# Second tile's rows loaded ahead, and some of the first tile's products moved to rows 64 to 127

## What is computed

```
w   = softmax(weight_gen) over 7 taps, for each token and each of 8 heads
x1  = sum over 7 taps of w[k] * x[token - 6 + k]       (24 channels to a head)
h1  = x1 @ w_in1 (192 x 2048);   x2 = (max(h1, 0) * h1) @ w_out1 (2048 x 192)
h2  = x2 @ w_in2 (192 x 2048);   out = (h2 * cos(h2)) @ w_out2 (2048 x 192)
```

## Time and profile before

| | value |
|---|---|
| median of three runs | 1176.63 us |
| the profiled execution | 1176.54 us |
| its span, first to last instruction | 1174.7 us |
| TensorE busy | 1167.3 us (99%) |
| VectorE busy | 961.2 us (82%) |
| ScalarE busy | 805.9 us (69%) |
| GpSimd busy | 367.1 us (31%) |
| mean granted TensorE clock | 0.999 of full speed |

### The profile page before, as it was taken

The page is one execution under the profiler, slowest core; times in us unless marked ns, Lnnn a source line. Parts: engine busy times, 40 slices in busy tenths (PEclk is TensorE's granted clock), DMA queues, the critical chain, the costliest instruction groups (busy, mean ns, idle before and its releaser), DMA issues.

```text
span 1174.7 us, 25693 instructions
## 1 busy us (share of the span) xinstructions
PE 1167.3 (99%) x9906; PEld 1129.7 (96%) x9906; DVE 961.2 (82%) x1505; ACT 805.9 (69%) x1467; POOL 367.1 (31%) x265
## 2 busy tenths in 40 slices
PE   9999999999999999999999999999999999999998
PEld 7989999999999999999999999999999999999987
DVE  7968898878778787887878878787787878878787
ACT  5977766666666676666766666676666766666676
POOL 4994634070420606025070430705215070000000
PEclk9999999999999999999999999999999999999999
DMA  8511111110111101111011111101111000100001
GB/s 212 138 48 31 37 27 35 25 35 10 23 35 29 35 11 18 35 28 35 15 24 29 25 35 28 35 9 21 35 29 35 13 17 3 26 2 15 1 1 28
DMA packets 113173, 37.32 MB, mean 32 GB/s; under 512 B 101662, under 2 KB 110878, under 8 KB 113052
## 3 DMA queue, kind: packets, MB, share of 16 engines
q1 hardware_dynamic: 111100, 34.87, 14.3%
q10 hardware_dynamic: 1952, 0.80, 0.3%
HBM read 23.84 MB, written 6.29 MB: 26 GB/s over the span
## 4 chain that ended last, share of the span: by engine, by line
PE 99%; DVE 0%; ACT 0%; ACTq 0%; issue 0%
PE y L608 51%; PE h L608 46%; PE y L713 1%; PE h L637 0%; ACT L1131 0%; PE h L630 0%; PE y L674 0%; DVE tap L1426 0%; PE h L644 0%; PE h L640 0%; ACTq L378 0%; ACTq L389 0%; ACTq L433 0%; PE y L676 0%; PE y L675 0%
## 5 line engine op out<-in xcount | busy, mean ns | idle before, releaser
L608 PE MATMUL y<-g_hi,wo 64*128 64x512 f32 x3048 | 695.1, 393 | 0.2
L608 PE MATMUL y<-g_lo,wo 64*128 64x512 f32 x2032 | 515.9, 391 | 0.0
L608 PEld LDWEIGHTS y<-g_hi,wo 64*128 64x128 f32 x3048 | 414.3, 184 | 14.1 <-PE y L608 1.1
L529 POOL TENSOR_TENSOR tap<-xc,gen 128x768 f32<-128x768 f32 x98 | 151.3, 1550 | 575.4 <-DVE xd_lo L1513 555.3
L608 PEld LDWEIGHTS y<-g_lo,wo 64*128 64x128 f32 x2032 | 298.6, 184 | 1.7
L1167 ACT ACTIVATE turns<-turns 128x512 f32<-128x512 f32 x238 | 150.2, 631 | 182.6 <-DVE turns L1464 182.6
L608 PE MATMUL h<-xa_hi,wa_hi 64*128 64x512 f32 x1018 | 267.6, 397 | 0.1
L608 PE MATMUL h<-xa_hi,wa_lo 64*128 64x512 f32 x1018 | 262.7, 391 | 0.0
L608 PE MATMUL h<-xa_lo,wa_hi 64*128 64x512 f32 x1018 | 262.3, 391 | 0.0
L1484 DVE TENSOR_TENSOR h<-h,turns 128x512 f32<-128x512 f32 x238 | 165.6, 696 | 114.7 <-ACT turns L1167 114.2
L1458 DVE SCALAR_TENSOR_TENSOR h<-h,relu 128x512 f32<-128x512 f32 x249 | 173.4, 696 | 56.5 <-ACT relu L1142 54.3
(11 more groups left out here) (124 smaller groups left out, 1076.0 us busy)
## 6 DMA issues: line engine op xcount, KB each, us to landing
xc<-in_x_dram SPq DMA_DIRECT2D x60, 240.0 KB
out_dram<-arena SPq DMA_DIRECT2D x62, 64.0 KB, 1.9
xt_a<-x_blocks SPq DMA_DIRECT2D x224, 16.0 KB, 1.8
arena<-in_moe_w_out_dram SPq DMA_DIRECT2D x16, 192.0 KB, 3.3
arena<-in_moe_w_in_dram SPq DMA_DIRECT2D x16, 128.0 KB, 2.6
out_dram<-arena SPq DMA_DIRECT2D x62, 32.0 KB, 1.7
xt_d<-x_blocks SPq DMA_DIRECT2D x112, 16.0 KB, 1.8
arena<-in_moe_w_in_dram SPq DMA_DIRECT2D x16, 64.0 KB, 2.9
```

The lines of the kernel that those rows point to most:

```text
L529: pool.tensor_tensor(tap[:, k % 2, :].rearrange("p (r g) -> p r g", g=GROUP), rows[k], wk, ALU.mult).then_inc(pool_step, 1)
L608: return pe.matmul(o, w[rows, :], x[rows, :], start=start, stop=stop)
```

## The change

Six things are edited:

1. SP's `load_rows(1)` stands ahead of `load_gen(sp, 1)`.
2. `CONV_SLOTS` moves the second tile's convolution up: three operations after slot 0, two after slot 1, one after each of slots 2 to 9. `turn_at(0)` goes from slot 13 to slot 12.
3. The three softmax steps that stood after slot 0 now stand ahead of the low parts of x, before slot 0.
4. SP copies the high part of the last 64 channels of x, and for pieces 3 to 7 the matching `wd_lo` and every second 128 columns of `wd_hi`, from rows 0 to 63 to rows 64 to 127, each by a DMA inside the on-chip memory.
5. In slots 6 to 15, `xd_hi*wd_lo` (even slots), or `xd_hi*wd_hi` and `xd_hi*wd_lo` (odd slots), is made on BOTTOM. An even slot then has 10 products on TOP and 9 on BOTTOM, an odd one 9 and 10.
6. In all of slots 3 to 19 the first BOTTOM `up_a` is issued ahead of the first TOP `down_a`, and the last TOP `down_a` is the slot's last product.

```
-        return (SLOTS - 3, SLOTS - 9)[t] if t < PEEL else TURN
+        return (SLOTS - 4, SLOTS - 9)[t] if t < PEEL else TURN
-        CONV_SLOTS = (1, 1, 2, 2, 3, 4, 5, 6, 7, 8, 9, 10, 11)
+        CONV_SLOTS = (0, 0, 0, 1, 1, 2, 3, 4, 5, 6, 7, 8, 9)
-        SOFTMAX_AFTER = {0: [(1, 2), (1, 3), (1, 4)]}
-        SOFTMAX_AFTER.update({n: [(n - 1, 0)] for n in range(3, 10)})
+        SOFTMAX_AFTER = {n: [(n - 1, 0)] for n in range(3, 10)}
+        def moved_down(n):
+            return () if not FIRST_MOVED * PF <= n < SLOTS else (0, 1) if n % 2 else (1,)
...
+            def copy_head_weights(pc):
+                cols, odd = slice(pc * PIECE, (pc + 1) * PIECE), slice(pc * PIECE + P, (pc + 1) * PIECE)
+                sp.wait_ge(piece_ready[pc], 2)
+                for w, at in ((wd_lo, cols), (wd_hi, odd)):
+                    sp.dma_start(w[DD:P, at].bitcast(F32), w[0:DD, at].bitcast(F32)).then_inc(head_w_copied[pc], 16)
...
+            load_rows(1)
             load_gen(sp, 1)
-            load_rows(1)
             for pc in range(RING, RING + 2):
                 load_piece(pc)
+            sp.wait_ge(x1_hi_ready, 2)
+            sp.dma_start(xd_hi[DD:P, 0, :].bitcast(F32), xd_hi[0:DD, 0, :].bitcast(F32)).then_inc(head_x_copied, 16)
             load_gen(sp, 2)
             for pc in range(RING + 2, PL + 4):
                 load_piece(pc)
+                if FIRST_MOVED <= pc - RING + 1 < PL:
+                    copy_head_weights(pc - RING + 1)
...
+            def up_d_bottom(o, f, k, **group):
+                w = wd_lo if k == 1 else wd_hi
+                return half(o, w[:, f * P:(f + 1) * P], xd_hi[:, 0, :], BOTTOM, **group)
...
                 for k in range(3):
                     last = down_a(down, BOTTOM, k, start=k == 0)
-                    last_up = up_d(o, 0, i, par, k)
+                    if k < len(kept):
+                        last_up = up_d(o, 0, i, par, kept[k])
...
+                pe.wait_ge(h1_left, n - HEAD_D1 + 1)
+                up_a(o, 0, i, par, BOTTOM, 0)
                 pe.wait_ge(y1_a_left, downs_in_halves(down_of_slot(n)))
                 down_a(down, TOP, 0)
-                pe.wait_ge(h1_left, n - HEAD_D1 + 1)
-                up_a(o, 0, i, par, BOTTOM, 0)
+                up_a(o, 0, i, par, BOTTOM, 1)
                 down_a(down, TOP, 1)
-                up_a(o, 0, i, par, BOTTOM, 1)
+                last_up = up_a(o, 0, i, par, BOTTOM, 2, stop=not moved)
+                if moved:
+                    pe.wait_ge(head_x_copied, 16)
+                    pe.wait_ge(head_w_copied[i // PF], 32)
+                for k in moved:
+                    last_up = up_d_bottom(o, i, k, stop=k == moved[-1])
+                last_up.then_inc(up1_done, 1)
                 down_a(down, TOP, 2, stop=True).then_inc(down1_done, 1)
-                up_a(o, 0, i, par, BOTTOM, 2, stop=True).then_inc(up1_done, 1)
...
                               ALU.subtract).then_inc(piece_ready[0], 1)
+            for op in range(2, 5):
+                softmax(1, op)
             for part in range(2):
                 dve.wait_ge(x1_hi_ready, part + 1)
```

More of the change, by code:

```diff
@@ L241, in conv_ffn_ffn_kernel @@
         w_copied = sem("w_copied")
+        head_w_copied = [sem(f"head_w_copied{pc}") for pc in range(PL)]
+        head_x_copied = sem("head_x_copied")
         y1_summed = sem("y1_summed")
@@ L250, in conv_ffn_ffn_kernel @@
         LATE = 4
+        FIRST_MOVED = 3
         ACT_SQUARES = (2, 3, 4, 5, 6, 7, 8)
-        CONV_SLOTS = (1, 1, 2, 2, 3, 4, 5, 6, 7, 8, 9, 10, 11)
+        CONV_SLOTS = (0, 0, 0, 1, 1, 2, 3, 4, 5, 6, 7, 8, 9)
         HI_AT = {4: 2, 5: 4, 6: 5, 7: 6, 8: 8, 9: 9, 10: 11, 11: 13, 12: 15, 13: 18, 14: 20, 15: 22}
@@ L1057, in head_slot @@
                 n = SLOTS * t + i
+                moved = moved_down(n)
+                kept = [k for k in range(3) if k not in moved]
                 ups_of_slot(t, i, n, -1)
```

## The result

The changed kernel took **1183.35 us** (median of 6, 1180.97 to 1184.53), the kernel before, beside it, 1176.62 (6 runs, 1176.37 to 1177.24): ratio 1.0054, 95% interval 1.0043 to 1.0065. It is slower by 6.7 us; the forecast was 1176.3, with an upper end of 1177.8. The profiled execution is its fastest, 1180.97 us, span 1179.2, 4.5 us over the span before.

The account below looks back on a forecast made before the run. TensorE held 99% of the chain, with TOP bounding a head slot and VectorE close to the bound up to slot 6. 2.87 + 0.10 - 3.34 = -0.37 us gave 1176.3 us, range 1174.4 to 1177.8.

Parts of the forecast that it names:

- the softmax steps ahead of slot 0: VectorE before x's low parts: scaling step takes one turn behind POOL, x 1.17 us later, TensorE's third product about 1.15.
- Convolution after slots 0 and 1: VectorE's three operations after slot 0 and two after slot 1 delay TensorE; slot 6 starts 2.87 us late, x's delay included.
- Products moved: Slots 6 to 15: TOP loses 15 products, 3.50 us, less 0.16 for lags; gain 3.34 us.
- after slot 16 all follows TensorE: Past the faster slots, everything was taken to shift along with TensorE, carrying the sum of -0.37 us to the end.
- nearly 9 us on: SP's weight copies: first pair due about 35.5, nearly 9 us after POOL makes piece 3's wd_lo; counted 0.
- the rows' order: SP issues the second tile's rows before the softmax inputs: no wait taken, bounds 0 and 0.5 us.
- third rival: Pieces 4 and 5 arrive late, ScalarE waits 2.3 us before relu 3: +1.9 us, 1178.5 (1179.1 with upper delay); chance 0.06.
- the new order in slots 3 to 5: BOTTOM's first up_a earlier, TOP's down_a last: hidden behind TOP, taken as 0, else about 0.1 us a slot.
- ScalarE behind faster slots: Slots 6 to 9: ScalarE falls back 1.1 us against a reserve of about 1.3; cost 0.1 us, bounds 0 and 0.5.
- The second rival (program order): Matmuls start in program order, a pair of slots takes 20.4 products, gain only 1.87 us: +1.1, 1177.7; chance 0.15.
- The first rival: Early stall short: scaling step gets in ahead of POOL, few convolution meetings, delay 0.98 us: -2.3, 1174.4; chance 0.17.

Follow-up runs that it names:

- POOL held: Changed kernel with POOL waiting for the second tile's scaling step before its second operation (wd_lo of piece 1): 1176.67 us, ratio 0.9998.
- the two other kernels whose profiles show 3.54 and 3.57: Kernel before with only the softmax steps ahead of x, 1184.55 us; changed kernel with eight fillers instead of one before slot 0's third product, 1181.62 us.
- the run with 0.83: Kernel before with the products moved, their copies and new order, plus POOL's wait for x2_split before the third tile's second convolution product: 1176.12 us, ratio 0.9992.

## Why the prediction was wrong

**The failed step is the softmax steps ahead of slot 0.** It saw the meeting with POOL, but priced it as one turn: "the later one ends its own time less 0.12 after the other", 18.38, x 1.17 late. In the profiled execution x was 1.74 late (18.87 against 17.13), and added to the kernel before the step stood 3.54 us. The rule came from meetings at 24.22 and 26.67. The trace of before has POOL's operations from 17.37 to 21.04, six of them, each starting before the recorded end of the one ahead; that list was in reach and wasn't counted. But it doesn't settle the price by itself. At 22.38 the same step, beside such a stream, took 0.39; it got in between these two operations of POOL, and the second of them took 0.89 instead of 0.74:

```profile
22.06 0.46 POOL L566 TENSOR_TENSOR wo<-arena,wo 128x128 fp32r<-128x128 f32 x1
22.48 0.89 POOL L568 TENSOR_TENSOR wo<-arena,wo 128x256 fp32r<-128x256 f32 x1
```

The Trainium skill, "SBUF — State Buffer", section "Who interferes with whom", calls the pair of ports that both engines share an exclusive lock. The runs agree that one holds the other off; a bound of one instruction, as the prediction used, is not what they show.

**And a term was missing: the clock.** The text said what was late next but never asked what TensorE's pause does to its clock. After the pause of 1.47 us the granted clock was 0.50 for ten microseconds. With POOL held the pause is 0.47 us, the clock stays 1.00, and the time is 6.7 us shorter. That POOL holding off the scaling step starts all of this is shown by that one wait; that the pause's length brings the clock down is not: it also fell behind a pause of 0.67 us, with POOL held and no product moved. The runs separate the pause and the clock only roughly: against the run with POOL held the third product is 0.98 us late, and slot 4 4.03 (31.46 against 27.43). The difference of 3.0 is what the slow stretch adds, against a run in which TensorE itself waits 1.24 us for VectorE there. How much of the step from 1180.97 to 1183.35 between executions is a longer wait of the scaling step stays open; the two other kernels whose profiles show 3.54 and 3.57 make it likely.

**Convolution after slots 0 and 1: right in mechanism, a little too dear.** Counted at 2.54 at slot 4 and 2.87 at slot 6, together with x's 1.17; with POOL held it is 2.15 at slot 4, with x 0.77 late, and 2.14 at slot 6 (32.63 against 30.49). Without x's share that is 1.37 counted and 1.38 measured at slot 4, but 1.70 and 1.37 at slot 6: slot 1's product was counted with a turn behind POOL, 1.45 us, and took 1.02.

**Products moved: the size was off, and the path to the end.** Counted 3.34; the five pairs give 2.67 together. An even slot takes 2.42 us instead of 2.33, an odd one 2.20 instead of 2.10 to 2.17. The trace shows most of that on TOP, where the first `down_a` now follows right behind BOTTOM's last one: the next product starts 0.33 us after it and not 0.23 (42.82 to 43.15, and 45.02 to 45.36). The prediction counted such a longer step for BOTTOM only. The medians give 2.4 where an early delay stands ahead, but only 0.2 by themselves, 0.85 with the x2 meeting avoided, and neither of these two is clear of the noise. The prediction's "after slot 16 all follows TensorE" failed: POOL runs by its own list, so moving TensorE against it made one new meeting (x2's low part, 0.69 to 2.05 us) and stretched one wait (ScalarE for the shift, 0.89 to 1.99).

**The copies: "nearly 9 us on" failed.** The cover held only under the late slots. With these on time the recorded waits for the first pair were 0.39 to 2.16 us: in the run with 0.83 its second copy was issued at 27.01 and wanted by 32.75, behind four softmax inputs and a piece that SP had issued since 22.69.

**Right:** the rows' order costs nothing (third rival refuted, 1176.66; ScalarE waited 0.46 us for piece 4 instead of 0.37); the new order in slots 3 to 5 shows no loss (2.57 and 2.64 us for slots 4 and 5 with the products moved alone, as before). The 0.10 us for ScalarE behind faster slots was not measured by itself.

**Luck.** With POOL held the kernel took 1176.67, close to the forecast of 1176.3. That doesn't bear out the sum: the delay was counted 0.7 too long, the moved products 0.7 too high, and these two errors largely cancel.

**The second rival (program order)** is refuted as a mechanism: it asked for 20.4 products a pair, 4.75 us, with the odd slot at 2.4, and it took 4.63 and 4.62, with the odd slot at 2.20. The starts say so directly: in slot 9 TOP's last product starts at 45.59 and BOTTOM's last moved product, ahead of it in the program, at 45.83. That the time came out slower has another cause. **The first rival**, the step getting in ahead of POOL, never occurred by itself; the start was 0.32 us behind POOL's operation, not 0.03. Where a wait made it so, slot 4 was still 2.15 late, not 0.98.

## What to carry to other kernels

Before an operation of VectorE with two inputs in the on-chip memory goes to a new place ahead of a gate, list POOL's operations from that point to its next real gap, not only the one beside it. Take that whole stretch as the upper end of the meeting's price, and add what TensorE's clock can do behind the pause. A wait on POOL that lets the gating operation pass costs little, and was worth 6.7 us here. And where TensorE gets faster while another engine runs by a fixed list, look for the first place where its in-order neighbours wait for that list. Several such waits can stand one behind the other, and here a gain of over a microsecond showed only when they went together.

## What the runs showed of the hardware that was not expected

- POOL operations without a gap kept a VectorE scaling step waiting for six of them (3.54 and 3.57 us against 0.39), and a 128x32 TENSOR_SCALAR with one input from 18.82 to 21.10 (0.22 at 21.74 in the kernel before, 0.52 at 16.73 in the changed one); each got in at POOL's first gap of 0.14 us. In the changed kernel's profiled execution the same step got in between two operations that overlap by 0.04 us in the record, and the POOL operation behind it took 0.96 instead of 0.73. What decides between the two is not settled.
- A pause of 1.47 us on TensorE, with long work before and after, was followed by ten microseconds at the lower level; one of 2.48 us, at 28.87 in the run with the steps behind x, was not: the clock stayed 1.00. And one of 0.67 us, with POOL held and no product moved, was followed by slow products from 20.15 to 26.76, where one of 0.47 us in the same place was not. So the pause's length alone doesn't decide, and here a pause under a microsecond was no guard against it.
